# A two-block feed-forward kernel: the second block's first product as seven block products, its weights and their sums prepared in DRAM, its slopes on GpSimd

## The chip, the cores and the metric

One core of one Trainium2 chip. The metric is the device time of one execution in microseconds (us). The engines are called PE (TensorE), DVE (VectorE), ACT (ScalarE), POOL (GpSimd) and SP (SyncE, which only issues transfers here).

## The reference

```python
X = np.fft.fft(np.fft.fft(x, axis=1), axis=2).real        # x: 2 x 3008 x 256
x = X.reshape(6016, 256)
h = x @ w_in                                               # 256 -> 2048
g = np.where(h > 0, h, np.exp(np.minimum(h, 0)) - 1)
x = g @ w_out                                              # 2048 -> 256
h = x @ w_in2                                              # second block, 256 -> 2048
g = np.maximum(h, 0) + alpha * np.minimum(h, 0)            # alpha: one slope per feature
return g @ w_out2                                          # 2048 -> 256
```

## The kernel before

Every product of the two blocks is made of three matmuls in fp32r: each operand is split into a high part and a low rest, and high x high, high x low and low x high are added up in PSUM.

Tokens run in NT = 6 tiles of up to 1024 columns, a plus half of TW = 512 and a minus half of 512 (384 in the last tile). The 2048 hidden features run in NF = 16 slices of 128. A step is one slice of one tile; there are S1 = 96 steps in each block, and PE interleaves two jobs in each: the up product of step s and the down product of step s - 3.

- First block: `up1` is 7 matmuls (the Fourier transform is folded into the weights W1). ACT copies one half (`copy_q`), DVE combines the halves into H (`combine`, two instructions), ACT and DVE form the activation (`neg`, `exp_neg`, `elu`), ACT rounds it to Gh (`g_hi`, L481), DVE takes the rest Gl (`g_lo`, L625). `down1` is 12 matmuls into ACC, which holds the four output blocks in four PSUM banks. In the middle of tiles 0 to 4, `flip2` makes the inputs of the next tile.
- Between the blocks the result of each tile goes to DRAM (`y_scratch`) and comes back as `y_in`, which is split into `y_hl`, for tile 0 by ACT and DVE in four pieces at slices 9 to 12 of the first block's last tile.
- Second block: `up2` (L380 to L382) is 12 matmuls: 2 input blocks of 128, times the plus and the minus half, times three. ACT takes the positive part and the negated negative part from PSUM (`second`, L542 and L544), DVE adds the slope times the negative part (`prelu`, L617), then `g_hi` (L483), `g_lo` (L627) and the 12 matmuls of `down`. At slice 2 of each tile ACT and DVE copy the last tile's ACC out.

Everything is written out by hand: each engine's list is in program order and waits on semaphores. PE's up product of step s waits until the PSUM half of step s - 2 has been read, and its down product for `lo_ready`, which DVE's `g_lo` gives.

POOL splits the weights. Each piece of 512 columns is loaded to `raw`, its high part is one `tensor_scalar` (L265), its rest one `tensor_tensor` (L266). W2's 8 pieces run at the start; the 8 pieces of W3 and 8 of W4 (the second block's weights) wait for the last `flip2` (their place is T1's) and then for one `down_done` each, so they run beside the last tiles of the first block:

```python
if k > after_w2:
    gp.wait_ge(down_done, NF * (LAST - 1) + FLIP_AT - 2 + W34_PACE * (k - after_w2))
```

Of the kernel before, what the change touches and what calls it, by code (L numbers as in the profile page):

```python
# [8 lines left out]
PT = 128  # L9
# [28 lines left out]
def program(nc, x, wa, wb, w2, w3, w4, alpha, c47, cw, cf, out):  # L38
# [4 lines left out]
    y_dram = nc.dram_tensor("y_scratch", [NT, PT, YW], fp32).ap()  # L43

# [13 lines left out]
    y_hl = at("y_hl", o1, [PT, 2 * 2 * YW], f32r)  # L58
    W1_HALF = 2 * YW // (4 * PT)
# [4 lines left out]
    W4 = at("W4", o2, [PT, 2, NF * D], f32r)  # L64
    W3h = at("W3h", o2 + 32 * KB, [PT, ND * F], f32r)
# [19 lines left out]
    W3l = at("W3l", o5, [PT, ND * F], f32r)  # L85
# [9 lines left out]
    with ExitStack() as ctx:  # L95
# [14 lines left out]
        w34_ready = sem("w34_ready")  # L110
# [10 lines left out]
        half_done = sem("half_done")  # L121
        y0h_ready, yh_ready, yl_ready = sem("y0h_ready"), sem("yh_ready"), sem("yl_ready")
# [19 lines left out]
        def _(sp):  # L142
# [68 lines left out]
        def _(gp):  # L211
            n = [0]

            def chain(ins):
                n[0] += 1
                ins.then_inc(pool_step, 1)
                gp.wait_ge(pool_step, n[0])
# [12 lines left out]
            gp.wait_ge(alpha_in, 16)  # L230
            chain(gp.tensor_scalar(nalpha[:, :], alpha_sb[:, :], -1.0, 0.0, ALU.mult, ALU.add))

            pieces = []

            def add(src, hi, lo):
                for c in range(src.shape[1] // 512):
                    sl = slice(c * 512, (c + 1) * 512)
                    pieces.append((src[:, sl], hi[:, sl], lo[:, sl]))

            add(w2, W2[:, 0, :], W2[:, 1, :])  # L240
            after_w2 = len(pieces)
            add(w3, W3h, W3l)
            add(w4, W4[:, 0, :], W4[:, 1, :])

            def load(k):
                gp.dma_start(raw[:, k % 2, :], pieces[k][0]).then_inc(raw_in[k % 2], 16)

            gp.wait_ge(f1_done, 2 * 6)
            load(0)
            load(1)  # L250
# [8 lines left out]
            for k, (_, hi, lo) in enumerate(pieces):  # L259
                if k == after_w2:  # L260
                    gp.wait_ge(f2_done, NT)
                if k > after_w2:
                    gp.wait_ge(down_done, NF * (LAST - 1) + FLIP_AT - 2 + W34_PACE * (k - after_w2))
                gp.wait_ge(raw_in[k % 2], 16 * (k // 2 + 1))
                chain(gp.tensor_scalar(hi, raw[:, k % 2, :], 1.0, 0.0, ALU.mult, ALU.add))  # L265
                ins = gp.tensor_tensor(lo, raw[:, k % 2, :], f32(hi), ALU.subtract)  # L266
                ready = w2_ready if k < after_w2 else w34_ready
                ins.then_inc(ready, 1)
                gp.wait_ge(ready, k + 1 if k < after_w2 else k + 1 - after_w2)
                if k + 2 < len(pieces):  # L270
                    load(k + 2)

        @block.tensor
        def _(pe):
# [87 lines left out]
            def up2(t, f, m):  # L362
                s = NF * t + f
                j = f % 2
                if f == 0:
                    pe.wait_ge(yl_ready, 2 * t + 2)
                if s < 2:
                    pe.wait_ge(comb_ready, S1 + s - 1)
                else:
                    pe.wait_ge(act_ready, S1 + s - 1)  # L370

                def mov(hl, k, w):
                    o = t % 2 * 2 * YW + hl * YW + k * TW
                    return y_hl[:, o:o + w]

                for sign, w in ((0, TW), (1, m)):
                    o = PQ[:, j, sign * TW:sign * TW + w]
                    for c in range(ND):
                        sl = slice(c * F + f * PT, c * F + (f + 1) * PT)
                        mm(o, W3h[:, sl], mov(0, sign * ND + c, w), start=c == 0, stop=False)  # L380
                        mm(o, W3h[:, sl], mov(1, sign * ND + c, w), start=False, stop=False)  # L381
                        ins = mm(o, W3l[:, sl], mov(0, sign * ND + c, w), start=False, stop=c == ND - 1)  # L382
                ins.then_inc(up_done, 1)

            def down(s, W):
# [6 lines left out]
                for d in range(ND):  # L392
                    sl = slice(f * D + d * PT, f * D + (d + 1) * PT)
                    for sign, w in ((0, TW), (1, m)):
                        o = ACC[:, sign * ND + d, 0:w]
                        c = sign * TW
                        mm(o, W[:, 0, sl], Gh[:, j, c:c + w], start=f == 0, stop=False)  # L397
                        mm(o, W[:, 0, sl], Gl[:, j, c:c + w], start=False, stop=False)  # L398
                    for sign, w in ((0, TW), (1, m)):
                        o = ACC[:, sign * ND + d, 0:w]  # L400
                        c = sign * TW
                        ins = mm(o, W[:, 1, sl], Gh[:, j, c:c + w], start=False, stop=f == NF - 1)  # L402
                    if s == 2 * S1 - 1 and d < ND - 1:
                        ins.then_inc(half_done, 1)
                ins.then_inc(down_done, 1)

            def down1(s):
                if s < NF and s % 2 == 0:
                    pe.wait_ge(w2_ready, s // 2 + 1)
                down(s, W2)  # L410

            def down2(s):
                down(s, W4)

# [12 lines left out]
            pe.wait_ge(w34_ready, 16)  # L427
            for f in range(3):
                up2(0, f, TW)
                down1(S1 - 3 + f)  # L430
            for s in range(3, S1):
                up2(s // NF, s % NF, width(s) - TW)
                down2(S1 + s - 3)
            for s in range(S1 - 3, S1):
                down2(S1 + s)

        @block.scalar
        def _(act):
# [36 lines left out]
            def g_hi(s, bias):  # L475
                j, n = s % 2, width(s)
# [27 lines left out]
            def y0_split_hi(k):  # L504
                act.wait_ge(y_loaded, 16)
                act.wait_ge(up_done, S1 - NF + W1_HALF)
                fn(y_hl[:, k * TW:(k + 1) * TW], y_in[:, k * TW:(k + 1) * TW], ACT.Copy).then_inc(y0h_ready, 1)

            eo_hi(0)
            copy_q(0)  # L510
            for s in range(S1):
# [13 lines left out]
                if t == LAST and f in SPLIT_AT:  # L525
                    y0_split_hi(SPLIT_AT.index(f))

            def y_split_hi(t, half):
                c = half * ND * TW
                m = TW - SKIP if t == LAST and half else TW  # L530
                if half == 0:
                    act.wait_ge(y_loaded, 16 * t + (32 if t == LAST else 16))
                o = t % 2 * 2 * YW + c
                dst = y_hl[:, o:o + ND * TW].rearrange("p (a b) -> p a b", a=ND)
                src = y_in[:, c:c + ND * TW].rearrange("p (a b) -> p a b", a=ND)
                fn(dst[:, :, 0:m], src[:, :, 0:m], ACT.Copy).then_inc(yh_ready, 1)

            def second(s):
                j, n = s % 2, width(s)
                act.wait_ge(up_done, s + 1)  # L540
                act.wait_ge(g_ready, s - 1)
                fn(H[:, j, 0:n], PQ[:, j, 0:n], ACT.Relu)  # L542
                act.wait_ge(lo_ready, s - 1)
                fn(G[:, j, 0:n], PQ[:, j, 0:n], ACT.Relu, scale=-1.0).then_inc(act_ready, 1)  # L544

            g_hi(S1 - 1, -1.0)
            for s in range(S1, 2 * S1):
                t, f = s // NF - NT, s % NF
                second(s)
                if s > S1:  # L550
                    g_hi(s - 1, None)
                if f in (6, 9) and t < LAST:
                    y_split_hi(t + 1, (f - 6) // 3)
                if f == 2:
                    y_plus(NT + t - 1)
# [7 lines left out]
        def _(dve):  # L563
# [72 lines left out]
            def y0_split_lo(k):  # L636
# [3 lines left out]
                if k % 2:  # L640
                    ins.then_inc(yl_ready, 1)
# [119 lines left out]
```

## Time and profile before

| | us |
|---|---|
| median of 3 runs | 1018.0 (1017.17 to 1018.95) |
| the profiled execution | 1018.47 |
| its span | 1016.7 |
| PE busy | 999.1 (98%) |
| ACT busy | 655.6 (64%) |
| DVE busy | 632.0 (62%) |
| POOL busy | 89.2 (9%) |

Matmul rows are pipelined: a row of 0.39 us starts while the one before it still runs, so PE's rate is read from the distance of the starts. The first block's steps run from about 58 us to 489 us of the span, the second's from there to the end.

### The profile page before, as it was taken

How to read it: one execution, taken by the hardware profiler on the slowest of the kernel's cores; microseconds unless marked ns; L12 is line 12 of the kernel's file. 1: busy time of each engine (PE TensorE's matmuls, PEld its weight loads, DVE VectorE, ACT ScalarE, POOL GpSimd, SP SyncE). 2: the span in 40 equal slices, each digit the busy share in tenths (PEclk: the TensorE clock that was granted, in tenths of full speed). 3: DMA queues.
4: the chain of work that ended last, by engine and by line, in shares of the span. 5: the costliest groups of instructions: out<-in, count | busy, mean ns of one | idle time of the engine just before them, and what ended most of it. 6: DMA issues, size and time to landing. Idle time of an engine off the chain costs nothing.

```text
span 1016.7 us, 11653 instructions
## 1 busy us (share of the span) xinstructions
PE 999.1 (98%) x4610; PEld 832.2 (82%) x4610; DVE 632.0 (62%) x640; ACT 655.6 (64%) x733; POOL 89.2 (9%) x95
## 2 busy tenths in 40 slices
PE   7979999999999999999999999999999999999997
PEld 6868888888888888878888888888888888888886
DVE  3357887887887887899645445445545545544443
ACT  2247887887787787778766566565555655565554
POOL 3370000000000005860000000000000000000000
PEclk9979999999999999999999999999999999999999
DMA  9420010010010010230020020010002002000101
GB/s 241 132 83 1 1 42 1 1 41 1 1 42 1 1 42 32 63 135 0 1 78 1 1 83 1 1 51 33 0 1 83 1 1 78 1 1 0 42 1 42
DMA packets 8482, 34.59 MB, mean 34 GB/s; under 512 B 1338, under 2 KB 2042, under 8 KB 6508
## 3 DMA queue, kind: packets, MB, share of 16 engines
q1 hardware_dynamic: 5612, 25.03, 7.4%
q0 software_dynamic: 2816, 8.82, 2.9%
q8 instruction: 36, 0.59, 0.2%
q14 instruction: 18, 0.15, 0.1%
HBM read 21.34 MB, written 12.48 MB: 33 GB/s over the span
## 4 chain that ended last, share of the span: by engine, by line
PE 59%; DVE 1%; ACT 0%; issue 0%; DVEq 0%; ACTq 0%
PE ACC L397 11%; PE ACC L402 10%; PE ACC L398 10%; PE PQ L382 8%; PE PQ L381 8%; PE PQ L380 8%; DVE Gl L625 1%; PE PQ L353 0%; PE PQ L354 0%; PE PQ L359 0%; PE PQ L355 0%; PE PQ L358 0%; PE PQ L360 0%; PE PQ L357 0%; DVE H L607 0%; DVE Gl L627 0%
## 5 line engine op out<-in xcount | busy, mean ns | idle before, releaser
L397 PE MATMUL ACC<-Gh,W 128*128 128x512 f32 (+1 forms) x768 | 298.7, 389 | 3.8 <-DVE Gl L625 2.8
L398 PE MATMUL ACC<-Gl,W 128*128 128x512 f32 (+1 forms) x768 | 297.0, 387 | 0.0
L627 DVE TENSOR_TENSOR Gl<-G,Gh 128x1024 fp32r<-128x1024 f32 (+1 forms) x96 | 115.5, 1203 | 214.6 <-ACT Gh L483 214.6
L402 PE MATMUL ACC<-Gh,W 128*128 128x512 f32 (+1 forms) x768 | 234.7, 387 | 0.0
L542 ACT ACTIVATE H<-PQ 128x1024 f32<-128x1024 f32 (+1 forms) x96 | 97.1, 1011 | 131.0 <-PE PQ L382 131.0
L397 PEld LDWEIGHTS ACC<-Gh,W 128*128 128x128 f32 x768 | 144.7, 188 | 38.1 <-issue 4.4
L398 PEld LDWEIGHTS ACC<-Gl,W 128*128 128x128 f32 x768 | 144.8, 188 | 28.0
L402 PEld LDWEIGHTS ACC<-Gh,W 128*128 128x128 f32 x768 | 144.0, 188 | 25.4
L483 ACT ACTIVATE Gh<-G 128x1024 fp32r<-128x1024 f32 (+1 forms) x96 | 100.1, 1042 | 75.2 <-PE ACC L402 71.5
L382 PE MATMUL PQ<-y_hl,W3l 128*128 128x512 f32 (+1 forms) x384 | 147.9, 385 | 0.0
L381 PE MATMUL PQ<-y_hl,W3h 128*128 128x512 f32 (+1 forms) x384 | 147.9, 385 | 0.0
L380 PE MATMUL PQ<-y_hl,W3h 128*128 128x512 f32 (+1 forms) x384 | 147.8, 385 | 0.0
L625 DVE SCALAR_TENSOR_TENSOR Gl<-G,Gh 128x1024 fp32r<-128x1024 f32 (+1 forms) x96 | 116.4, 1213 | 32.8 <-ACT Gh L481 32.4
L612 DVE SCALAR_TENSOR_TENSOR G<-H,G 128x1024 f32<-128x1024 f32 (+1 forms) x96 | 122.4, 1275 | 0.5 <-ACT G L502 0.5
L617 DVE SCALAR_TENSOR_TENSOR G<-G,nalpha,H 128x1024 f32<-128x1024 f32 (+1 forms) x96 | 120.7, 1257 | 0.7 <-ACT G L544 0.7
L473 ACT ACTIVATE Qs<-PQ 128x512 f32<-128x512 f32 x96 | 57.3, 597 | 83.2 <-PE PQ L355 83.2
L481 ACT ACTIVATE Gh<-G 128x1024 fp32r<-128x1024 f32 (+1 forms) x96 | 99.2, 1033 | 9.1 <-DVE G L612 6.6
L497 ACT ACTIVATE G<-H 128x1024 f32<-128x1024 f32 (+1 forms) x96 | 99.5, 1037 | 4.1 <-DVE Gl L625 3.4
L544 ACT ACTIVATE G<-PQ 128x1024 f32<-128x1024 f32 (+1 forms) x96 | 96.3, 1003 | 7.0 <-DVE Gl L627 7.0
L502 ACT ACTIVATE G<-G 128x1024 f32<-128x1024 f32 (+1 forms) x96 | 99.1, 1032 | 0.0
L606 DVE TENSOR_TENSOR H<-PQ,Qs 128x512 f32<-128x512 f32 x96 | 66.4, 692 | 40.2 <-PE PQ L360 37.3
L380 PEld LDWEIGHTS PQ<-y_hl,W3h 128*128 128x128 f32 x384 | 72.1, 188 | 14.6
(70 smaller groups left out, 922.5 us busy)
## 6 DMA issues: line engine op xcount, KB each, us to landing
xr<-in_x SPq DMA_DIRECT2D x16, 384.0 KB, 4.2
raw<-in_w POOLq DMA_DIRECT2D x24, 256.0 KB, 3.1
y_scratch<-y_st SPq DMA_DIRECT2D x5, 1024.0 KB, 3.9
y_in<-y_scratch SPq DMA_DIRECT2D x5, 1024.0 KB, 8.2
out_y<-y_st SPq DMA_DIRECT2D x5, 1024.0 KB, 5.8
wn<-in_wa POOLq DMA_DIRECT2D x4, 256.0 KB, 11.0
wn<-in_wb POOLq DMA_DIRECT2D x4, 256.0 KB, 11.7
out_y<-y_st SPq DMA_DIRECT2D x2, 512.0 KB, 3.3
```

Source lines behind the costliest of these rows:

```text
L380: mm(o, W3h[:, sl], mov(0, sign * ND + c, w), start=c == 0, stop=False)
L381: mm(o, W3h[:, sl], mov(1, sign * ND + c, w), start=False, stop=False)
L382: ins = mm(o, W3l[:, sl], mov(0, sign * ND + c, w), start=False, stop=c == ND - 1)
L397: mm(o, W[:, 0, sl], Gh[:, j, c:c + w], start=f == 0, stop=False)
L398: mm(o, W[:, 0, sl], Gl[:, j, c:c + w], start=False, stop=False)
L402: ins = mm(o, W[:, 1, sl], Gh[:, j, c:c + w], start=False, stop=f == NF - 1)
L483: fn(Gh[:, j, 0:n], G[:, j, 0:n], ACT.Copy).then_inc(hi_ready, 1)
L497: fn(G[:, j, 0:n], H[:, j, 0:n], ACT.Relu, scale=-1.0).then_inc(neg_ready, 1)
L612: stt(G[:, j, 0:n], H[:, j, 0:n], 0.0, G[:, j, 0:n], ALU.max, ALU.add).then_inc(g_ready, 1)
L617: stt(G[:, j, 0:n], G[:, j, 0:n], nalpha[:, f:f + 1], H[:, j, 0:n], ALU.mult, ALU.add).then_inc(g_ready, 1)
L625: stt(Gl[:, j, 0:n], G[:, j, 0:n], bias, f32(Gh[:, j, 0:n]), ALU.add, ALU.subtract).then_inc(lo_ready, 1)
L627: tt(Gl[:, j, 0:n], G[:, j, 0:n], f32(Gh[:, j, 0:n]), ALU.subtract).then_inc(lo_ready, 1)
```

## The change

The tile's input is seen as 2 x 2 blocks (two input blocks, plus and minus half) and the weights of two slices as a 2 x 2 block matrix, so the second block's up products of two slices are one 2 x 2 by 2 x 2 block product. Before, this was 8 block products of 3 matmuls; now it is 7 (Winograd's form), on sums and differences of blocks. A loop pass (`pair`) now handles two slices; there are 48 pairs.

- PE. `pair(n)` issues 7 `product`s (3 matmuls each) and 8 quarters of `down` (3 matmuls each) in a written order. The products are accumulated in three banks, and two partial sums travel: ACT copies bank_a into bank_b in PSUM (the seed), and bank_b twice into SBUF (`u2`, `u3`).
- ACT, per pair: the seed, `u2`, `u3` and two copies of results into H (c11, c21), 512 wide each, and two `g_hi`. Before: four 1024-wide activations and two `g_hi`.
- DVE, per pair: two 512-wide adds from PSUM and u2 or u3 into H (c22, c12), two `join`s (max(H,0) + G, 1024 wide) in place of two `prelu`s, two `g_lo`.
- POOL, per pair: two `slope`s, G = min(H, 0) * alpha, 1024 wide, which the joins wait for.
- The operands of later tiles (`YS`, seven of them, each in two parts): four differences and seven rests on DVE, seven high parts on ACT, spread over pairs 1 to 7 of the tile before; the whole `y_hl` split is gone. Tile 0's operands are made by POOL alone beside the last tile of the first block. ACC is copied out in four 512-wide pieces.
- The weights. POOL forms W3's four sums and seven splits for two pairs at a time (18 instructions of 512 columns, four times) and W4's splits (16), paced by `up_done` from step 4 of the first block on, 4 instructions to 3 steps, staged in SBUF and stored in DRAM (7 MB and 4 MB). After the last `flip2` they are loaded from DRAM, W3 and three slices of W4 by POOL's queue, the rest of W4 over W2 by SP's queue as W2's slices are done with.

```diff
+W3_FROM = 4
+W4_A = 3
+W4_CUTS = (3, 6, 10, 13, 16)
...
+            def pace():
+                gp.wait_ge(up_done, W3_FROM + steps[0] * 3 // 4)
+                steps[0] += 1
...
+                if u:
+                    gp.wait_ge(w3_stored, 16 * u)
+                pace()
+                chain(gp.tensor_tensor(f32(lo[4]), a21, a22, ALU.add))
...
+                for q, src in ((0, a11), (1, a12), (3, a22), (2, f32(lo[2])), (4, f32(lo[4])), (5, f32(lo[5])), (6, f32(lo[6]))):
+                    pace()
+                    chain(hi_of(hi[q], src))
+                    pace()
+                    chain(gp.tensor_tensor(lo[q], src, f32(hi[q]), ALU.subtract))
+                gp.dma_start(w3_dram[:, 2 * u:2 * u + 2, :, :, :], f32(stage[:, :, :, :, :])).then_inc(w3_stored, 16)
...
+            def parts0(q, src):
+                gp.wait_ge(up_done, NF * LAST + 2 * Y0_ORDER.index(q) + 2)
+                chain(hi_of(ys0(q, 0), src))
+                gp.tensor_tensor(ys0(q, 1), src, f32(ys0(q, 0)), ALU.subtract).then_inc(y0_ready, 1)
...
+            def slope(s):
...
+                if k == 0:
+                    gp.wait_ge(c21_ready, n + 1)
+                    gp.wait_ge(c22_ready, n + 1)
+                else:
+                    gp.wait_ge(c11_ready, n + 1)
+                    gp.wait_ge(c12_ready, n + 1)
+                gp.wait_ge(lo_ready, s - 1)
+                gp.tensor_scalar(G[:, k, 0:w], H[:, k, 0:w], 0.0, alpha_sb[:, f:f + 1], ALU.min, ALU.mult).then_inc(slope_ready, 1)
...
-            def up2(t, f, m):
...
+            def product(n, q, bank, w, start):
...
+                mm(o, w3(p, q, 0), hi, start=start, stop=False, skip_group_check=True)
+                mm(o, w3(p, q, 0), lo, start=False, stop=False, skip_group_check=True)
+                mm(o, w3(p, q, 1), hi, start=False, stop=True, skip_group_check=True).then_inc(p_done[q], 1)
...
+            def pair(n):
+                a, b = S1 + 2 * n - 3, S1 + 2 * n - 2
...
+                product(n, 0, bank_a, TW, True)
...
+                product(n, 4, bank_e(n), m, True)
+                down(a, 0)
+                down(a, 1)
+                pe.wait_ge(seed_ready, n + 1)
+                product(n, 5, bank_b, TW, False)
+                product(n, 1, bank_a, TW, False)
+                down(a, 2)
+                pe.wait_ge(u2_ready, n + 1)
+                product(n, 6, bank_b, TW, False)
+                down(a, 3)
+                down(b, 0)
+                pe.wait_ge(u3_ready, n + 1)
+                product(n, 3, bank_b, TW, False)
+                down(b, 1)
+                down(b, 2)
+                pe.wait_ge(c22_ready, n + 1)
+                product(n, 2, bank_e(n), m, False)
+                down(b, 3)
...
+            for n in range(NT * NP):                       # ACT
...
+                fn(bank_b, bank_a, ACT.Copy).then_inc(seed_ready, 1)
+                if n:
+                    g_hi(S1 + 2 * n - 2, None)
...
+                fn(u2[:, :], bank_b, ACT.Copy).then_inc(u2_ready, 1)
...
+                fn(H[:, 1, 0:TW], bank_a, ACT.Copy).then_inc(c11_ready, 1)
...
+                fn(u3[:, :], bank_b, ACT.Copy).then_inc(u3_ready, 1)
...
+                g_hi(S1 + 2 * n - 1, None if n else -1.0)
...
+                fn(H[:, 0, 0:TW], bank_b, ACT.Copy).then_inc(c21_ready, 1)
...
+                if n:                                      # DVE
+                    join(S1 + 2 * n - 1)
+                    g_lo(S1 + 2 * n - 2, None)
...
+                tt(H[:, 0, TW:TW + m], bank_e(n)[:, 0:m], u3[:, 0:m], ALU.add).then_inc(c22_ready, 1)
+                g_lo(S1 + 2 * n - 1, None if n else -1.0)
...
+                tt(H[:, 1, TW:TW + m], bank_e(n)[:, 0:m], u2[:, 0:m], ALU.add).then_inc(c12_ready, 1)
+                join(S1 + 2 * n)
```

(The comments ACT and DVE in the diff are added here to tell the two lists apart.)

## Rows read from the trace of the kernel before

**Rows 1.** The page's first part: busy time, share of the span, instructions of an engine.
```profile
PE 999.1 (98%) x4610; PEld 832.2 (82%) x4610; DVE 632.0 (62%) x640; ACT 655.6 (64%) x733; POOL 89.2 (9%) x95
```

**Rows 2.** The head of the chain that ended last: shares of the span.
```profile
PE 59%; DVE 1%; ACT 0%; issue 0%; DVEq 0%; ACTq 0%
```

**Rows 3.** Timeline of a first-block step: start us, duration us, engine, line, operation.
```profile
331.20 0.39 PE L353 MATMUL PQ<-EO,W 128*128 128x512 f32 x1
...
332.56 0.39 PE L360 MATMUL PQ<-EO,W1e 128*128 128x512 f32 x1
...
332.99 0.69 DVE L606 TENSOR_TENSOR H<-PQ,Qs 128x512 f32<-128x512 f32 x1 [0.33 <-PE PQ L360]
...
334.61 1.23 DVE L625 SCALAR_TENSOR_TENSOR Gl<-G,Gh 128x1024 fp32r<-128x1024 f32 x1 [0.33 <-ACT Gh L481]
...
335.51 0.39 PE L353 MATMUL PQ<-EO,W 128*128 128x512 f32 x1
```

**Rows 4.** Timeline of PE, second block, a full step's first matmul and the next step's.
```profile
614.10 0.39 PE L380 MATMUL PQ<-y_hl,W3h 128*128 128x512 f32 x1
...
619.54 0.39 PE L380 MATMUL PQ<-y_hl,W3h 128*128 128x512 f32 x1
```

**Rows 5.** Timeline of PE, last tile: first wide, first narrow, end of an up product.
```profile
998.68 0.40 PE L380 MATMUL PQ<-y_hl,W3h 128*128 128x512 f32 x1
...
1000.08 0.33 PE L380 MATMUL PQ<-y_hl,W3h 128*128 128x384 f32 x1
...
1001.13 0.39 PE L397 MATMUL ACC<-Gh,W 128*128 128x512 f32 x1
```

**Rows 6.** Groups by line: shapes and count, busy us, mean ns, idle before, releasers.
```profile
L627 DVE TENSOR_TENSOR Gl<-G,Gh 128x1024 fp32r<-128x1024 f32 (+1 forms) x96 | 115.5, 1203 | 214.6 <-ACT Gh L483 214.6
...
L483 ACT ACTIVATE Gh<-G 128x1024 fp32r<-128x1024 f32 (+1 forms) x96 | 100.1, 1042 | 75.2 <-PE ACC L402 71.5 <-DVE G L617 3.7
...
L612 DVE SCALAR_TENSOR_TENSOR G<-H,G 128x1024 f32<-128x1024 f32 (+1 forms) x96 | 122.4, 1275 | 0.5 <-ACT G L502 0.5
...
L473 ACT ACTIVATE Qs<-PQ 128x512 f32<-128x512 f32 x96 | 57.3, 597 | 83.2 <-PE PQ L355 83.2
```

**Rows 7.** Timeline of POOL at the start: a small, a one-input, a two-input instruction.
```profile
21.92 0.20 POOL L231 TENSOR_SCALAR nalpha<-alpha_sb 128x16 f32<-128x16 f32 x1 [11.91 <-DMA alpha_sb<-in_alpha]
...
48.62 0.61 POOL L265 TENSOR_SCALAR W<-raw 128x512 fp32r<-128x512 f32 x1
49.32 1.27 POOL L266 TENSOR_TENSOR W<-raw,W 128x512 fp32r<-128x512 f32 x1
```

**Rows 8.** Timeline in the first block's last tile: POOL, then DVE.
```profile
457.27 2.01 POOL L266 TENSOR_TENSOR W<-raw,W 128x512 fp32r<-128x512 f32 x1
...
458.04 2.18 DVE L612 SCALAR_TENSOR_TENSOR G<-H,G 128x896 f32<-128x896 f32 x1
...
462.43 1.08 DVE L612 SCALAR_TENSOR_TENSOR G<-H,G 128x896 f32<-128x896 f32 x1
```

**Rows 9.** Timeline of ACT there: `copy_q` once a step, the last without POOL.
```profile
457.47 0.57 ACT L473 ACTIVATE Qs<-PQ 128x512 f32<-128x512 f32 x1
461.96 0.58 ACT L473 ACTIVATE Qs<-PQ 128x512 f32<-128x512 f32 x1
466.04 0.60 ACT L473 ACTIVATE Qs<-PQ 128x512 f32<-128x512 f32 x1 [0.69 <-PE PQ L355]
```

**Rows 10.** Timeline where the blocks meet: first second-block matmul, last `exp_neg`.
```profile
489.61 0.40 PE L380 MATMUL PQ<-y_hl,W3h 128*128 128x512 f32 x1
...
491.73 0.94 ACT L502 ACTIVATE G<-G 128x896 f32<-128x896 f32 x1
```

**Rows 11.** Timeline of the end: last `g_lo` and the down product behind it.
```profile
1008.02 1.09 DVE L627 TENSOR_TENSOR Gl<-G,Gh 128x896 fp32r<-128x896 f32 x1 [1.02 <-ACT Gh L483]
...
1009.17 0.50 PE L397 MATMUL ACC<-Gh,W 128*128 128x512 f32 x1 [0.43 <-DVE Gl L627]
```

**Rows 12.** Transfers: issues, KB each, median us from issue to landing.
```profile
y_in<-y_scratch SPq DMA_DIRECT2D x5, 1024.0 KB, 8.2
```

More of the change, by code:

```diff
@@ L229, in _, with load_w2 @@
             chain(gp.memset(f32(W1e[:, :]), 0.0))
[L230 to L246, printed above, removed]
+            W2_LOADS = NF * D // 512
+            def load_w2(k):
+                gp.dma_start(raw[:, k % 2, :], w2[:, k * 512:(k + 1) * 512]).then_inc(raw_in[k % 2], 16)
             gp.wait_ge(f1_done, 2 * 6)
-            load(0)
-            load(1)
+            load_w2(0)
+            load_w2(1)
             gp.wait_ge(w1l_ready, 8)
@@ L257, in _, with hi_of @@
             gp.memset(f32(W1[0:1, :, 2:4, :]), 0.0).then_inc(w1_ready, 1)
[L259 to L263, printed above, removed]
-                gp.wait_ge(raw_in[k % 2], 16 * (k // 2 + 1))
[L265 to L271, printed above, removed]
+            def hi_of(dst, src):
+                return gp.tensor_scalar(dst, src, 1.0, 0.0, ALU.mult, ALU.add)
@@ new lines, in _ @@
+            for k in range(W2_LOADS):
+                gp.wait_ge(raw_in[k % 2], 16 * (k // 2 + 1))
+                src = raw[:, k % 2, :].rearrange("p (f d) -> p f d", d=D)
+                fs = slice(2 * k, 2 * k + 2)
+                chain(hi_of(W2[:, fs, 0, :], src))
+                gp.tensor_tensor(W2[:, fs, 1, :], src, f32(W2[:, fs, 0, :]), ALU.subtract).then_inc(w2_ready, 1)
+                gp.wait_ge(w2_ready, k + 1)
+                if k + 2 < W2_LOADS:
+                    load_w2(k + 2)
@@ new lines, in _ @@
+            gp.wait_ge(w3_stored, 16 * NP // 2)
+            for v in range(4):
+                for j in range(2):
+                    o = (2 * v + j) * 512
+                    gp.dma_start(raw[:, j, :], w4_in[:, o:o + 512]).then_inc(raw_in[j], 16)
+                loads += 1
+                if v:
+                    gp.wait_ge(w4_stored, 16 * v)
+                for j in range(2):
+                    gp.wait_ge(raw_in[j], 16 * loads)
+                    src = raw[:, j, :].rearrange("p (f d) -> p f d", d=D)
+                    pace()
+                    chain(hi_of(stage4[:, 2 * j:2 * j + 2, 0, :], src))
+                    pace()
+                    chain(gp.tensor_tensor(stage4[:, 2 * j:2 * j + 2, 1, :], src, f32(stage4[:, 2 * j:2 * j + 2, 0, :]), ALU.subtract))
+                gp.dma_start(w4_dram[:, 4 * v:4 * v + 4, :, :], f32(stage4[:, :, :, :])).then_inc(w4_stored, 16)
@@ new lines, in _, with ys0 @@
+            gp.wait_ge(f2_done, NT)
+            for n in range(3):
+                gp.dma_start(f32(W3a[:, 2 * n:2 * n + 2, :, :, :]), w3_dram[:, 2 * n:2 * n + 2, :, :, :]).then_inc(w3_loaded[n], 16)
+            gp.wait_ge(w4_stored, 64)
+            gp.dma_start(f32(W4a[:, :, :, :]), w4_dram[:, 0:W4_A, :, :]).then_inc(w4a_loaded, 16)
+            gp.dma_start(f32(W3b[:, :, :, :, :]), w3_dram[:, NP - 2:NP, :, :, :]).then_inc(w3_loaded[3], 16)
+            def ys0(q, part):
+                return YS[0][q][:, part, :]
@@ new lines, in sum0 @@
+            def sum0(q, a, b):
+                gp.wait_ge(up_done, NF * LAST + 2 * Y0_ORDER.index(q) + 2)
+                chain(gp.tensor_tensor(YT[0][q][:, :], a, b, ALU.subtract))
+            def parts0(q, src):
+                gp.wait_ge(up_done, NF * LAST + 2 * Y0_ORDER.index(q) + 2)
+                chain(hi_of(ys0(q, 0), src))
+                gp.tensor_tensor(ys0(q, 1), src, f32(ys0(q, 0)), ALU.subtract).then_inc(y0_ready, 1)
+            gp.wait_ge(y_loaded, 16)
+            parts0(0, y_block(1, 1))
@@ L360, in up1, with down1 @@
                 mm(o, W1e[:, f * PT:(f + 1) * PT], eo(t, 4), start=False, stop=True).then_inc(up_done, 1)
-            def up2(t, f, m):
[L363 to L385, printed above, removed]
+            def product(n, q, bank, w, start):
+                t, p = n // NP, n % NP
+                if p == 0:
+                    if t:
+                        pe.wait_ge(ysl_ready, NQ7 * (t - 1) + YS_ORDER.index(q) + 1)
+                    else:
+                        pe.wait_ge(y0_ready, Y0_ORDER.index(q) + 1)
+                hi, lo = YS[t % 2][q][:, 0, 0:w], YS[t % 2][q][:, 1, 0:w]
+                o = bank[:, 0:w]
+                mm(o, w3(p, q, 0), hi, start=start, stop=False, skip_group_check=True)
+                mm(o, w3(p, q, 0), lo, start=False, stop=False, skip_group_check=True)
+                mm(o, w3(p, q, 1), hi, start=False, stop=True, skip_group_check=True).then_inc(p_done[q], 1)
+            def down1(s):
+                if s < NF and s % 2 == 0:
+                    pe.wait_ge(w2_ready, s // 2 + 1)
                 f, j = s % NF, s % 2
@@ L401, in down @@
                         c = sign * TW
-                        ins = mm(o, W[:, 1, sl], Gh[:, j, c:c + w], start=False, stop=f == NF - 1)
-                    if s == 2 * S1 - 1 and d < ND - 1:
-                        ins.then_inc(half_done, 1)
+                        ins = mm(o, W2[:, f, 1, sl], Gh[:, j, c:c + w], start=False, stop=f == NF - 1)
                 ins.then_inc(down_done, 1)
[L407 to L410, printed above, removed]
@@ L412, in down2, with down @@
-            def down2(s):
-                down(s, W4)
+            def down(s, g):
+                j, d, sign = s % 2, g // 2, g % 2
+                if g == 0:
+                    pe.wait_ge(lo_ready, s + 1)
+                if s < S1:
+                    W, first, last, w = W2[:, s % NF, :, :], False, s == S1 - 1, (TW, WL - TW)[sign]
+                else:
+                    n, i = (s - S1) // 2, (s - S1) % NF
+                    f = 2 * (n % NP) + 1 - i % 2
+                    W, first, last, w = w4_slice(f), i == 0, i == NF - 1, (TW, minus(n))[sign]
+                    if n < NP and g == 0 and f < W4_A:
+                        pe.wait_ge(w4a_loaded, 16)
+                    if n < NP and g == 0 and f >= W4_A:
+                        pe.wait_ge(w4_loaded[[f < c for c in W4_CUTS[1:]].index(True)], 16)
+                    if first and sign == 0:
+                        pe.wait_ge(accp_ready, 2 * (n // NP) + d + 1)
+                    if first and sign == 1:
+                        pe.wait_ge(accm_ready, 2 * (n // NP) + d + 1)
+                c = sign * TW
+                o = ACC[:, sign * ND + d, 0:w]
+                sl = slice(d * PT, (d + 1) * PT)
+                mm(o, W[:, 0, sl], Gh[:, j, c:c + w], start=first, stop=False)
+                mm(o, W[:, 0, sl], Gl[:, j, c:c + w], start=False, stop=False)
+                ins = mm(o, W[:, 1, sl], Gh[:, j, c:c + w], start=False, stop=last)
+                if g == 3:
+                    ins.then_inc(down_done, 1)
+                elif last:
+                    ins.then_inc(acc_done, 1)
@@ L426, in _ @@
                     down1(s - 3)
[L427 to L435, printed above, removed]
+            for n in range(NT * NP):
+                pair(n)
+            for s in range(2 * S1 - 3, 2 * S1):
+                for g in range(4):
+                    down(s, g)
         @block.scalar
@@ L538, in second, with acc_plus @@
[L538 to L555, printed above, removed]
+            def acc_plus(n, d):
+                act.wait_ge(acc_done, 3 * (n - NT + 1) + 2 * d + 1)
+                act.wait_ge(y_stored, y_free(n))
+                fn(y_st[:, 0, d, :], ACC[:, d, :], ACT.Copy).then_inc(accp_ready, 1)
@@ L556, in _ @@
+            g_hi(2 * S1 - 2, None)
             g_hi(2 * S1 - 1, None)
-            act.wait_ge(y_stored, y_free(2 * NT - 1))
             for d in range(ND):
-                act.wait_ge(half_done, 1) if d < ND - 1 else act.wait_ge(down_done, 2 * S1)
-                fn(y_st[:, 0, d, :], ACC[:, d, :], ACT.Copy).then_inc(yp_ready, 1)
+                acc_plus(2 * NT - 1, d)
         @block.vector
```

294 lines of the change are left out of this document (216 added, 78 removed).

## The prediction

> **What bounds the kernel now.** I read the page's busy shares first: PE is busy for 98% of the span, ACT and DVE for under two thirds [rows 1]. A pipelined matmul counts as busy, so this alone could hide a slow rhythm. The chain that ended last says the same from the other side: its named work is PE's, 59% (the pieces of the pipelined matmuls), against 1% of DVE [rows 2]. Third, the timeline: a second-block step starts 5.44 us after the one before, for 24 matmuls of 512 columns, 0.2267 us each [rows 4]; in the last tile an up product's 6 wide matmuls take 1.40 us and its 6 narrow ones 1.05, so 0.233 and 0.175 each [rows 5]. A first-block step takes 4.31 us for 19 matmuls, again 0.2267 [rows 3]. PE's matmul count is the bound in both blocks, so each matmul that goes is worth its 0.2267 us, as long as the other engines keep up.
>
> **What goes.** A pair of slices took 48 matmuls and takes 45. In five tiles that is 40 pairs x 3 x 0.2267 = 27.2 us. In the last tile a pair had 24 wide and 24 narrow matmuls, 9.79 us; five of the seven products are now wide, so it has 27 and 18, 9.44 us: 0.35 x 8 = 2.8 us. Together 30.0 us.
> POOL's old W3 and W4 splits go from the first block's last tile. There a step took 4.49 us beside them and 4.08 once they had ended [rows 9]: DVE's `elu` needed 2.18 us in place of 1.08, and POOL's rest 2.01 in place of 1.27 [rows 7, 8]. Five such steps: 2.0 us back. The ACT and DVE split of tile 0 also goes; those steps ran at 4.08, so nothing.
>
> **Does a pair run at PE's rate?** This is the choice that decides. I lay a full pair out by durations of rows. PE has 15 groups of 0.68 us, 10.2 us in all. A group's last result is seen by another engine 0.88 us after the group's start: 2 x 0.2267, then 0.39, then 0.04 [rows 3]. A 512-wide ACT copy takes 0.60, `g_hi` 1.04, `g_lo` 1.20 [rows 6]; an add from PSUM 0.69 [rows 3]; a join is `elu`'s form, 1.22 without POOL (1.275 on average, rows 6). `slope` is in no row. A one-input POOL instruction takes 0.61 for 512 columns and 0.20 for 16 [rows 7], so 1.04 for 1024; with two inputs 1.27, so (1.27 - 0.20) x 2 + 0.20 = 2.34. These are its ends; it has one tensor input, so I take 1.04.
> - P0 is done at 0.9, the seed at 1.5; P5 needs it at 2.72. P5 is done at 3.6, u2 at 4.2; P6 needs it at 4.76. P1 is done at 4.3, c11 at 4.9. P6 at 5.6, u3 at 6.25; P3 needs it at 6.8. c22 at 7.0; P2 needs its bank at 8.84. P3 at 7.7, c21 at 8.3. The least margin is 0.5 us.
> - The long way round: P2 is done at 9.72. c12 ends at 10.4; the join of k = 0 runs to 11.5, since its slope ended near 9.6 (it waits for c21 and for `g_lo` to leave); the slope of k = 1 can read only behind that join, to 12.6; the join of k = 1 to 13.8; `g_lo` of k = 0 to 15.0. PE wants it at group 9 of the next pair, 10.2 + 6.1 = 16.3. Margin 1.2 us.
> ACT has 3.0 + 2.1 = 5.1 us of work and DVE 2.4 + 2.4 + 1.4 = 6.2, of 10.2. The seven operands of the next tile add at most three 0.69 us instructions to one pair; DVE then reaches c22 near 7.5, done by 8.2, before 8.84. So nothing here costs, and 30 us stand.
> What I took from rows here is that DVE and POOL exclude each other: the row at 458.04 has `elu` waiting for the whole of POOL's `tensor_tensor` [rows 8]. The Trainium skill (SBUF — State Buffer, section "Who interferes with whom") calls this an exclusive lock between a DVE instruction with two SBUF inputs and a GpSimd one that reads SBUF; the trace agrees (2.18 us against 1.08). By a reading without it the slope would run beside the join and the margin would be 2.2 us, with the same sum.
>
> **What the new form adds.**
> - POOL's 88 instructions in the first block (44 in the sums and rests of W3 with two inputs, 28 with one, 16 for W4), 4 to 3 steps, mean 1.0 us. They wait for `up_done`, which also starts `combine`, an instruction pair with one SBUF input, 1.3 us, with 0.33 us idle behind it [rows 3]. A single one of 1.27 fits into 1.6 us. Two in a row (every third step) overrun by 0.4 us, two with two inputs by 1.0; DVE idles 0.66 us per step, and `g_lo` ends 1.2 us before PE's next down product (334.61 + 1.23 against 335.51 + 1.6), so PE does not see it. After the eight stores POOL is behind and runs without its pacing; a few steps may cost 0.4 each, as in rows 9. I take 1 us, between -1 (nothing was lost before either) and 18 (the second rival).
> - Tile 0's operands on POOL: 18 instructions, 11 x 1.27 + 7 x 0.61 = 18 us over 14 steps, in four bursts of over 3 us. By 0.41 us for each burst: 1.5 us, between 0 and 5.
> - The seam. P5 of pair 0 needs the seed, which stands behind the last `exp_neg` on ACT: that ended at 492.67, the seed at 493.3, and P5 would be due at 489.61 + 2.6 = 492.2 [rows 10]. 1.1 us.
> - Tile ends. In a tile's second pair ACT has two more copies of 0.6 and DVE two of 0.69 and a difference; `g_lo` of k = 1 ends near 9.2, the last piece of ACC at 9.9, and PE wants that bank at group 14, 9.52. 0.4 us x 6 = 2.4, between 0 and 6.
> - The end. Behind the last pair the long way round has 2.45 us of down product (two wide quarters of 0.70, two narrow of 0.52) to hide it. In narrow durations (1.09 for `g_lo`, rows 11) it ends at 13.9 after a pair start, and PE is there at 9.44 + 2.45 = 11.9: 2.0 us idle, where 0.43 was idle before [rows 11]. 1.5 us.
> - Transfers: W3 and W4 come back as 11 MB after the last `flip2`. At 8.2 us for 1 MB [rows 12], which holds the latency too, that is 90 us for all of it, and the 8 MB on POOL's queue 66 us, from 387 to 453; the first pair starts at 489. Hidden behind tiles 4 and 5; if that cover failed, it would be a plain wait at 489.
> - `load_y` of tile 1 is queued on SP behind the last piece of W4, issued near 490. Both are 1.8 MB, 15 us, landed by 505; DVE asks for it in pair 1, near 507. Nothing, but 5 us if tile 0's operands come late: what is queued behind that DVE instruction is c22, for which PE waits.
>
> **Sum.** -30.0 - 2.0 + 1.0 + 1.5 + 1.1 + 2.4 + 1.5 = -24.5 us. The profiled execution of 1018.47 us (span 1016.7 and 1.8 around it) becomes 994.0; the median of the runs lies 0.5 lower: 993.5. I say 994.
>
> **The rivals.**
> - GpSimd becomes the bound, slower than before. If `slope` costs x, DVE's first join starts at 10.3 or at 8.6 + x, whichever is later, and the long way round ends x + 3.6 us after that. It is free up to x = 2.0. With the two-input price, x = 2.34, it ends at 16.9, 0.6 us late in each of 48 pairs: 29 us, 1023. From x = 2.3 on the change loses. For it: no row has a per-feature factor and a minimum on POOL. Against it: one tensor input, and the copy form had two operations as well. The Trainium skill speaks for it: GPSIMD Engine Reference, "Performance versus the Vector engine", gives 2.6 cycles at 1.2 GHz for each element of a two-input instruction, an estimate of 2.2 us for 1024, and advises against elementwise work there; its 1.8 cycles for a tight loop would be 1.5 us, which fits the margin. The row of 0.61 us for 512 is faster than either.
> - The first block falls out of step. In rows 9 a late POOL made DVE late, and DVE made the next POOL instruction late, for five steps. If that held over the 66 steps of the weight work, with 4/3 instead of 2 instructions a step, it costs 66 x 0.41 x 2/3 = 18 us: 1011. For it: DVE has 0.66 us a step to spare. Against it: beside the full tile 4 the old splits ran without loss, and `up_done` is a better moment than `down_done`.
> - The seams cost more: tile 0's operands and the load of tile 1 late, ACC's pieces late by 1 us. 5 + 1 + 4 us more: about 1003.
> - All additions are hidden: -30.0 - 2.0, 986.
>
> **How the numbers follow.** Forecast (989 to 999) 0.62; seams 0.12; first block out of step, wholly or in part (1000 to 1013), 0.12; everything hidden 0.06; GpSimd's slope between free and decisive (1000 to 1016) 0.02, deciding 0.06. A measurement of this kernel tells from no change only what is over 0.2%, 2 us. Faster is all but the last and some of the worst mixes: 0.90; within 0.2% 0.03; slower 0.07. The range reaches from 988, near the hidden case, to 1009, into the second rival, and leaves out about 2 in 10.
>
> **What will show it.** PE: 4466 matmuls; second-block pairs 10.2 us apart, 9.44 in the last tile; a wider distance names the rival, and the idle time before PE's products and downs says which way round was late. POOL: `slope` near 1.04 us. First block: step distances of 4.31 us between 75 and 430 us of the span, and the first product at 489.6 give or take 2 us. Seams: PE idle once near 492, six times about 0.4, and 2 us before the last but one down product. The prediction is wrong if pairs are over 10.4 us apart or if the second block starts after 500.

## The result and the profile after

The change made the kernel slower: 1161.5 us (median of 4 runs, 1158.8 to 1166.0) against 1017.6 (the kernel before, now with a fourth run), a ratio of 1.142 (95% interval 1.1385 to 1.1456). I had said 994.

The page's first part and its slices of POOL's busy tenths and of PE's granted clock, after the change; the span is 1160.2 us:

```profile
PE 1023.8 (88%) x4466; PEld 826.0 (71%) x4466; DVE 712.6 (61%) x783; ACT 606.9 (52%) x808; POOL 563.7 (49%) x278
...
POOL 3461313123155006256666666665566666565563
PEclk9999999999999999989999998989999989899898
```

The head of the chain that ended last:

```profile
POOL 24%; PE 24%; DVE 9%; issue 8%; ACT 1%; POOLq 0%; DVEq 0%; ACTq 0%
```

PE issues the 4466 matmuls that were forecast, 144 fewer than in [rows 1], yet its busy share fell from 98% to 88%, and POOL now has as large a part (24%) as PE of a chain that was PE's [rows 2]. The groups by line name the instruction (columns as in rows 6):

```profile
L424 POOL TENSOR_SCALAR G<-H,alpha_sb 128x1024 f32<-128x1024 f32 (+1 forms) x96 | 407.1, 4249 | 262.5 <-ACT H L767 222.8 <-DVE H L931 34.7 <-DVE Gl L852 4.8
...
L842 DVE SCALAR_TENSOR_TENSOR G<-H,G 128x1024 f32<-128x1024 f32 (+1 forms) x96 | 115.5, 1203 | 239.5 <-POOL G L424 239.2
L582 PE MATMUL ACC<-Gh,W 128*128 128x512 f32 x324 | 139.9, 432 | 101.2 <-DVE Gl L852 101.2
```

Read upward: PE's down product waits 101 us for `g_lo`, the joins wait 239 us for `slope`, and one `slope` takes 4.25 us on average. One loop in the timeline, ACT, POOL, DVE and PE merged from it by me in order of start (a POOL row that merges the two slopes stands first, the second slope alone behind it):

```profile
716.38 0.60 ACT L767 ACTIVATE H<-PQ 128x512 f32<-128x512 f32 x1 [2.03 <-PE PQ L536]
...
717.07 8.53 POOL L424 TENSOR_SCALAR G<-H,alpha_sb 128x1024 f32<-128x1024 f32 x2 [6.11 <-ACT H L767]
...
720.81 1.23 DVE L842 SCALAR_TENSOR_TENSOR G<-H,G 128x1024 f32<-128x1024 f32 x1
720.86 4.75 POOL L424 TENSOR_SCALAR G<-H,alpha_sb 128x1024 f32<-128x1024 f32 x1
...
725.64 1.23 DVE L842 SCALAR_TENSOR_TENSOR G<-H,G 128x1024 f32<-128x1024 f32 x1 [3.60 <-POOL G L424]
726.78 1.22 DVE L852 TENSOR_TENSOR Gl<-G,Gh 128x1024 fp32r<-128x1024 f32 x1
...
728.05 0.50 PE L582 MATMUL ACC<-Gh,W4a 128*128 128x512 f32 x1 [1.26 <-DVE Gl L852]
```

The second slope starts 3.79 us behind the first; a slope that waits for nothing reads 3.71 us. The second one reads 4.75: it waits about 1.05 us for the first join, which starts beside it. The same holds in all 48 pairs (4.75 to 4.77 us in the full tiles). This is the long way round of the prediction, with another price for one of its steps. The seeds' starts (one seed in each pair) lie 13.62 us apart on average over the second block (640.4 us for 47 distances), where 10.2 was forecast, and 9.44 in the last tile.

The first block went as forecast in its steps, not in its end. Steps stayed at 4.31 us; its last tile ran at 4.08 with three steps of 4.60, 4.43 and 4.60 beside tile 0's operands (1.4 us; I had 1.5), and the five slow steps of [rows 9] are gone. The second block began at 485.0 us, which lies outside the 489.6 give or take 2 that I had named; in the later runs of the same first block it began between 484.5 and 489.5. Most of the difference arises at the very start: the first four steps took 13.7 us here and 16.1 in e1 below, whose first block is the same code.

### The profile page after: what moved, and what is told of

Its sections match the earlier page's. It is cut to its first block, busy times and chain, and to the rows that moved or that the text cites. A ratio compares the mean times of both kernels' runs of the same rounds, so it can differ in the third digit from the quotient of the medians.

```text
span 1160.2 us, 12203 instructions
## 1 busy us (share of the span) xinstructions
PE 1023.8 (88%) x4466; PEld 826.0 (71%) x4466; DVE 712.6 (61%) x783; ACT 606.9 (52%) x808; POOL 563.7 (49%) x278
## 4 chain that ended last, share of the span: by engine, by line
POOL 24%; PE 24%; DVE 9%; issue 8%; ACT 1%; POOLq 0%; DVEq 0%; ACTq 0%
POOL G L424 24%; DVE Gl L852 5%; PE ACC L582 4%; PE ACC L583 3%; PE ACC L584 3%; PE PQ L536 2%; PE PQ L534 2%; PE PQ L535 2%; DVE H L936 2%; PE ACC L552 1%; PE ACC L557 1%; PE ACC L553 1%; DVE Gl L850 1%; DVE YS L892 0%; ACT H L767 0%
## 5 line engine op out<-in xcount | busy, mean ns | idle before, releaser
L424 POOL TENSOR_SCALAR G<-H,alpha_sb 128x1024 f32<-128x1024 f32 (+1 forms) x96 | 407.1, 4249 | 262.5 <-ACT H L767 222.8
L842 DVE SCALAR_TENSOR_TENSOR G<-H,G 128x1024 f32<-128x1024 f32 (+1 forms) x96 | 115.5, 1203 | 239.5 <-POOL G L424 239.2
L582 PE MATMUL ACC<-Gh,W 128*128 128x512 f32 x324 | 139.9, 432 | 101.2 <-DVE Gl L852 101.2
L582 PEld LDWEIGHTS ACC<-Gh,W 128*128 128x128 f32 x324 | 66.6, 206 | 130.7 <-DVE Gl L852 118.5
L552 PE MATMUL ACC<-Gh,W 128*128 128x512 f32 x372 | 145.5, 391 | 3.5 <-DVE Gl L850 3.5
L553 PE MATMUL ACC<-Gl,W 128*128 128x512 f32 x372 | 144.4, 388 | 0.0
L850 DVE SCALAR_TENSOR_TENSOR Gl<-G,Gh 128x1024 fp32r<-128x1024 f32 (+1 forms) x96 | 120.0, 1250 | 28.5 <-ACT Gh L688 27.9
L583 PE MATMUL ACC<-Gl,W 128*128 128x512 f32 x324 | 134.0, 414 | 0.0
L584 PE MATMUL ACC<-Gh,W 128*128 128x512 f32 x324 | 133.7, 413 | 0.0
L837 DVE SCALAR_TENSOR_TENSOR G<-H,G 128x1024 f32<-128x1024 f32 (+1 forms) x96 | 123.7, 1288 | 0.6 <-ACT G L709 0.6
L557 PE MATMUL ACC<-Gh,W 128*128 128x512 f32 x372 | 113.9, 387 | 0.0
L534 PE MATMUL PQ<-YS,W3a 128*128 128x512 f32 (+1 forms) x252 | 104.3, 414 | 8.1 <-ACT u L754 7.0
L757 ACT ACTIVATE H<-PQ 128x512 f32<-128x512 f32 x48 | 28.7, 597 | 141.6 <-DVE G L842 141.5
L535 PE MATMUL PQ<-YS,W3a 128*128 128x512 f32 (+1 forms) x252 | 101.9, 404 | 0.0
L536 PE MATMUL PQ<-YS,W3a 128*128 128x512 f32 (+1 forms) x252 | 101.7, 404 | 0.0
L746 ACT ACTIVATE PQ<-PQ 128x512 f32<-128x512 f32 x48 | 27.9, 582 | 128.9 <-PE PQ L536 128.9
```

The lines of the kernel that those rows point to most:

```text
L424: gp.tensor_scalar(G[:, k, 0:w], H[:, k, 0:w], 0.0, alpha_sb[:, f:f + 1], ALU.min, ALU.mult).then_inc(slope_ready, 1)
L534: mm(o, w3(p, q, 0), hi, start=start, stop=False, skip_group_check=True)
L535: mm(o, w3(p, q, 0), lo, start=False, stop=False, skip_group_check=True)
L536: mm(o, w3(p, q, 1), hi, start=False, stop=True, skip_group_check=True).then_inc(p_done[q], 1)
L552: mm(o, W2[:, f, 0, sl], Gh[:, j, c:c + w], start=f == 0, stop=False)
L553: mm(o, W2[:, f, 0, sl], Gl[:, j, c:c + w], start=False, stop=False)
```

## The experiments

The first four ask what makes the slope slow, and what the kernel is without it. e1 to e3 edit one line of the changed kernel; e4 takes `slope` off POOL and changes `join`. In the cuts below G and H stand for G[:, k, 0:w] and H[:, k, 0:w], and the semaphore at the end of a line is left out; where only a + line is shown, its - line is that of e1. A time without a ratio is that of a single run; the changed kernel's four runs spread over 7 us.

**e1_const**, a constant for the factor:
```diff
-gp.tensor_scalar(G, H, 0.0, alpha_sb[:, f:f + 1], ALU.min, ALU.mult)
+gp.tensor_scalar(G, H, 0.0, 0.15, ALU.min, ALU.mult)
```


> The changed kernel with the slope's per-feature factor replaced by one constant, 0.15 (the slopes are then not the reference's); minimum and multiplication stay. Theory A, the minimum is what makes the slope 4.25 us: it stays near 4.25 us, pairs near 13.8 us apart, time near 1160. Theory B, the factor read from SBUF makes it: the slope falls to 1.0 to 1.5 us, pairs to 10.2 us, time near 989 (second block from 485.0, 40 x 10.2 + 8 x 9.44, 1.1 + 2.4 + 1.5 of seams, 13.3 of end, 1.8 outside the span). Theory C, the slope waits for DVE's lock or is slow wherever it stands: near 4.25 us here and in the two kernels beside it.

1088.9 us, pairs 12.07 apart. The slope still takes 3.6 us, so B falls as the main cause. The time fell by 73 us all the same; e12 and what follows it take that up.

**e2_ptr**, the factor without the minimum:
```diff
+gp.tensor_scalar(G, H, alpha_sb[:, f:f + 1], 0.0, ALU.mult, ALU.add)
```


> The changed kernel with the slope as H times the per-feature factor plus 0, no minimum (so positive values are counted with their slope too; not the reference's activation). Theory A: the slope falls to 1.0 to 1.5 us, pairs 10.2 us apart, time near 989. Theory B: it stays near 4.25 us, time near 1160. Theory C: 4.25 us.

989.7 us, pairs 10.20. A holds: it is the minimum. (Mean 1.61 us per slope, waits for DVE in it.)

**e3_muladd**, neither:
```diff
+gp.tensor_scalar(G, H, 0.15, 0.0, ALU.mult, ALU.add)
```


> The changed kernel with the slope as H times 0.15 plus 0: no minimum, no factor from SBUF, the form of POOL's copies (not the reference's activation). Theories A and B: 1.0 to 1.1 us (0.61 for 512 columns), pairs 10.2 us apart, time near 989. Theory C: 4.25 us. If A and B both hold a part, this one alone is fast and the other two lie between.

988.5 us. C falls: the place in the program and the waits for DVE cost nothing in PE's time. The seeds' 47 distances add up to 474.3 us against 640.4: 166.1 of the 173.5 us between the two spans (1160.2 and 986.7); the rest is the end, 9.6 longer, and a start 2.2 earlier.

**e4_dve**, the slope on DVE, inside the join:
```diff
-stt(G[:, k, 0:w], H[:, k, 0:w], 0.0, G[:, k, 0:w], ALU.max, ALU.add)
+stt(G[:, k, 0:w], H[:, k, 0:w], alpha_sb[:, f:f + 1], H[:, k, 0:w], ALU.mult, ALU.max)
```


> The changed kernel with no slope on POOL: DVE's join is one instruction, max(alpha x H, H), the same as the reference's for every slope up to 1. If POOL's slope alone cost the time (A, B or C), each pair keeps PE busy: 10.2 us apart, 9.44 in the last tile, time 986 to 990, ratio to before near 0.97. The rival, that the seven-product form has a second bound of its own (ACT's five copies, the seed, the pieces of ACC), says pairs of 10.6 us or more and 1005 or more.

987.7 us, ratio to before 0.9705 (0.9683 to 0.9727); pairs 10.20 and 9.41. No second bound shows: the pairs run at PE's rate. Its chain is PE's again:

```profile
PE 58%; DVE 2%; ACT 1%; issue 0%; DVEq 0%; ACTq 0%
```

The next four ask which minimum is slow: any, or one order of operations.

**e5_swap**, factor first:
```diff
+gp.tensor_scalar(G, H, alpha_sb[:, f:f + 1], 0.0, ALU.mult, ALU.min)
```


> The changed kernel with the slope's two operations in the other order: H times the per-feature factor first, then the minimum with 0. The same function. Theory A1, any minimum is slow on POOL: slope near 3.7 us and time near 1160. Theory A2, only a pair of operations whose first is not the multiplication is slow (the one fast form seen so far multiplies first): 1.1 us without waits, time near 989.

**e6_max**, a maximum:
```diff
+gp.tensor_scalar(G, H, 0.0, 0.15, ALU.max, ALU.mult)
```


> The changed kernel with a maximum with 0 in place of the minimum, and the constant 0.15 as factor (not the reference's slopes). A1, widened to comparisons: 3.6 us, time near 1089 as with the minimum and a constant. If only the minimum itself is slow: 1.1 us and 989.

**e7_addmul**, another order of two plain operations:
```diff
+gp.tensor_scalar(G, H, 0.0, 0.15, ALU.add, ALU.mult)
```


> The changed kernel with the slope as (H + 0) times 0.15: no comparison, the multiplication second (the minimum is left out). A1: 1.1 us without waits, time near 988. A2: 3.6 us, time near 1089.

**e8_minonly**, one operation:
```diff
+gp.tensor_scalar(G, H, 0.0, None, ALU.min)
```


> The changed kernel with only the minimum with 0 in the slope, one operation, no factor (so negative values count fully). A1: still about 3.6 us if the price is of the minimum, time near 1089; if the price is of a pair of unlike operations, 1.1 us and 988.

1143.1, 1086.4, 989.7 and 1014.4 us. A2 falls (e7 is fast, e5 slow), A1 holds, for the maximum too. A lone minimum lies between, which neither theory had: 2.77 us. e5 came out 17 us under the 1160 expected, with the same price for a slope; why is taken up behind e12. What in POOL makes a minimum dear, no run shows. Lines and instructions of 128 columns in the order after, e1, e3, e6, e8 (ns: least, median, largest; the least are the 896-wide ones, without waits):

```profile
L424 POOL TENSOR_SCALAR G<-H,alpha_sb x96: 3274/4376/4774, 494.3 to 1142.3; 128x1024 f32<-128x1024 f32 x80, 128x896 f32<-128x896 f32 x16
```
```profile
L424 POOL TENSOR_SCALAR G<-H x96: 3193/3628/4478, 498.0 to 1070.8; 128x1024 f32<-128x1024 f32 x80, 128x896 f32<-128x896 f32 x16
```
```profile
L424 POOL TENSOR_SCALAR G<-H x96: 952/1603/1909, 496.4 to 973.3; 128x1024 f32<-128x1024 f32 x80, 128x896 f32<-128x896 f32 x16
```
```profile
L424 POOL TENSOR_SCALAR G<-H x96: 3196/3626/4477, 495.4 to 1068.1; 128x1024 f32<-128x1024 f32 x80, 128x896 f32<-128x896 f32 x16
```
```profile
L424 POOL TENSOR_SCALAR G<-H x96: 2445/2772/3619, 498.7 to 997.1; 128x1024 f32<-128x1024 f32 x80, 128x896 f32<-128x896 f32 x16
```

So 896 columns take 0.95 us with multiply and add, 2.45 with a minimum alone, 3.19 with a minimum or maximum and a multiplication; the factor from SBUF adds 0.06 to 0.08 (e2 and the changed kernel).

**e9_twice** tests the schedule's margin, a plain slope done twice:
```diff
+chain(gp.tensor_scalar(G, H, 0.15, 0.0, ALU.mult, ALU.add))
+gp.tensor_scalar(G, H, 0.15, 0.0, ALU.mult, ALU.add)
```


> The kernel with H times 0.15 plus 0 as slope (no minimum, constant factor), each slope computed twice, the second after the first: one slope then takes about 2 x 1.07 + 0.1 = 2.24 us where it took 1.07. It tests the schedule of the prediction, by which a slope is free up to 2.0 us: the long way round ends at 10.84 + 2.24 + 3.6 = 16.7 against 16.3, 0.35 us late in each of 48 pairs, 17 us more than the single one's 988.5: about 1005, pairs 10.55 us apart. If the margin were wider than the schedule has it, 990 or less; if the lock made POOL lose more, above 1015.

999.4 us, 11 more than the single one, where about 17 more was expected. Most pairs stay at 10.2; two of each tile, those with three more DVE instructions for the next operands, take 11.0. The margin of plain pairs was wider than 16.7 against 16.3 said; that of the loaded ones was too small.

**e10_tail** swaps two calls at the end of e4:
```diff
-            join(2 * S1 - 1)
             g_lo(2 * S1 - 2, None)
+            join(2 * S1 - 1)
```


> The version with the slope in DVE's join, and behind the last pair the rest of k = 0 computed before the join of k = 1. PE's idle time before the last but one down product (0.85 us) should fall to nothing and that before the last one come in its place, at most 0.4: about 0.5 us less than the 987.7 of the version without, which a comparison of times can hardly tell. Ratio to before 0.970.

986.6 us, ratio 0.9709 (0.9684 to 0.9734). Not told apart from e4, and the idle time it was meant to take away stayed at 0.85 us, with 0.47 more before the last product: ACT's `g_hi` sets it, not DVE's order. My reason for it was wrong.

**e11_before_dve** is the control, the kernel before with e4's slope (ACT's two activations become one copy):
```diff
-fn(G[:, j, 0:n], PQ[:, j, 0:n], ACT.Relu, scale=-1.0)
...
+stt(G[:, j, 0:n], H[:, j, 0:n], alpha_sb[:, f:f + 1], H[:, j, 0:n], ALU.mult, ALU.max)
```


> The kernel before, eight block products, with only its slopes changed: ACT copies the up product to H in one instruction, DVE forms max(alpha x H, H). PE bound it already, so the same time as before within 0.2% (1015 to 1019); then the 29 us of the version with seven products and the slope on DVE are the products' and not the slope form's. If the slope form itself helped, under 1013.

1017.0 us, ratio 0.9999 (0.9985 to 1.0013). So the 29 us of e4 are not the slope form's; they belong to the seven products and what was moved with them.

**e12_warm** takes up what the slope's price leaves open. In full tiles, the first distance left out, pairs of the changed kernel came 11.8 to 16.4 us apart, e1's 12.0 to 13.0, for slopes whose prices differ by 0.08 us. Two stretches of the changed kernel, behind an idle time of 2.65 us and after (us; busy and count of PE, PEld, DVE, ACT, POOL; granted clock; DMA):

```profile
713.40:719.50 6.10, 6.08 (x14) 4.84 (x15) 1.92 (x2) 1.54 (x3) 2.43 (x1) 0.50 0.00 0
719.50:726.40 6.90, 6.90 (x31) 5.65 (x30) 2.68 (x3) 2.72 (x4) 6.02 (x2) 0.99 0.00 0
```

Granted clock 0.50 is TensorE's lower level, 1.2 GHz: 14 matmuls in 6.1 us, then 31 in 6.9. PE stood idle once in each pair, mostly for 1.3 to 2.65 us; the clock fell in 20 of the 47 distances between seeds, 78 us in all. In full tiles 17 such distances were 15.1 us on average and the other 22 were 13.0. e12 puts discarded matmuls into that idle time:

```diff
                 down(a, 3)
+                if n:
+                    pe.wait_ge(c12_ready, n)
+                    for _ in range(9):
+                        mm(bank_e(n + 1), w3(p, 0, 0), YS[t % 2][0][:, 0, 0:TW], start=True, stop=True, skip_group_check=True)
                 down(b, 0)
```


> The changed kernel with nine more matmuls in each pair, 2.04 us, into the bank that is free then, just ahead of the down product that waits for the slopes; their results are thrown away. In the changed kernel PE stood idle 2.65 us there and then ran its next 14 matmuls 0.43 us apart at a lower granted clock, and pairs came 13.3 to 15.9 us apart. If those idle times bring the clock down and the clock draws the pairs out, PE now runs at full clock, all pairs take the 13.3 us of the slopes' loop (13.0 to 13.6), and the kernel is faster with more work: about 1140 (40 pairs x 0.5 less), granted clock 0.99. If the spread of the pairs comes from the slopes and DVE's lock alone, the time stays within 1150 to 1165. If the nine matmuls are simply in the way, above 1165.

1144.9 us, 14 us under the least of the four runs of the changed kernel (1158.8), with 423 more matmuls. Its span of 1143.1 has clock 0.995 and, in full tiles, distances of 13.27 to 14.30, 13.29 in most pairs. All 48 second slopes wait for the join here too, so the clock is what differs. From 500 to 900 us, the changed kernel first:

```profile
500.00:900.00 400.00, 326.55 (x1289) 253.28 (x1289) 203.49 (x223) 155.44 (x237) 248.95 (x58) 0.94 0.05 19
```
```profile
500.00:900.00 400.00, 375.15 (x1587) 292.46 (x1585) 207.11 (x227) 158.23 (x243) 256.26 (x59) 1.00 0.05 19
```

What it leaves is 13.29 against e1's 12.04. With the constant, the join is the one that waits, and reads 2.05 us:

```profile
650.57 3.63 POOL L424 TENSOR_SCALAR G<-H 128x1024 f32<-128x1024 f32 x1
650.64 2.05 DVE L842 SCALAR_TENSOR_TENSOR G<-H,G 128x1024 f32<-128x1024 f32 x1 [1.61 <-POOL G L424]
```

The slopes then run back to back and 1.07 us fewer stand in the loop. Who waits can't be read from which row starts first: in e1 and in 45 pairs of the changed kernel alike the slope's row starts ahead, by 0.06 to 0.07 us and by 0.05 to 0.06. e5 has both outcomes in one execution, here a pair of each:

```profile
558.47 3.71 POOL L424 TENSOR_SCALAR G<-H,alpha_sb 128x1024 f32<-128x1024 f32 x1
558.53 2.13 DVE L842 SCALAR_TENSOR_TENSOR G<-H,G 128x1024 f32<-128x1024 f32 x1 [0.30 <-POOL G L424]
...
544.96 4.77 POOL L424 TENSOR_SCALAR G<-H,alpha_sb 128x1024 f32<-128x1024 f32 x1
545.01 1.23 DVE L842 SCALAR_TENSOR_TENSOR G<-H,G 128x1024 f32<-128x1024 f32 x1 [2.67 <-POOL G L424]
```

From one first slope to the next, its eleven full loops of the first kind took 12.20 to 12.35 us, its 28 of the second kind 13.27 or more. In the changed kernel all 48 pairs are of the second kind, in e1 all of the first. That, and the clock at its lower level for 52 us in place of 78, sets e5 apart from the changed kernel and accounts for the 17 us. In the first kind the join waits only 0.9 us and ends while the slope still runs.

So an estimate splits the 166.1 us in four parts, which add up to 167: 93 with e1's price and order (567.3 - 474.3), 7.5 from the factor (0.16 x 47), 50 from the order (1.07 x 47), 16.5 from the clock (640.4 - 623.9, e12's sum).

## Why the prediction was wrong

- *The failed step* is the price of `slope`, "so 1.04 for 1024", with 2.34 as its other end. It measured 3.71 us without waits, 3.79 from its start to the next one's. I took the price from two rows of POOL that multiply and add, and bounded it by the number of inputs; the operation itself, a minimum, was in no row, and my upper end did not cover it. I wrote that no row had "a per-feature factor and a minimum", and gave the case 8%.
- *The mechanism was there*, as the first rival: POOL's slopes, the joins and `g_lo` hold up PE's down product. Its formula is not borne out. It puts a join between the two slopes of every pair, so that the loop is 6.1 + 2x us. With x = 3.79 that is 13.7 a pair, 3.5 us late, 167 us in 48 pairs: 1161, as measured. That this fits is in part luck. It is 13.29 in plain pairs at full clock (e12), and the lower clock, which I had not thought of, gives back about as much. And where the join is the one that waits, the formula is 1.3 us a pair too long: for e1's 3.63 it says 1146 (1088.9 measured), for e8's 2.77 it says 1063 (1014.4). The measured plain loops of e8 and e1, 10.4 and 12.04, are 4.8 + 2x. So "From x = 2.3 on the change loses" is wrong too: at 2.77 the kernel took 1014.4 us against 1017.0 before.
- *PE's rate*: right. Pairs of 10.20 and 9.41 wherever the slope is short (e2, e3, e4). The sum, made for such a slope, was 994.0; e3's profiled execution took 988.5, at the low edge of the range, near the case in which everything is hidden (986). By the sum the second block would begin at 490.1; in e3 it began at 487.2, which is 2.9 of the 5.5 us.
- *The additions*: POOL's weight work cost nothing (1.0 forecast; W3's instructions are 256 columns wide, 0.41 and 0.74 us, and not 512, as the section on the change says and the prediction prices). The seam measured 0.82 us (1.1), tile ends 0.2 each, in e3 and e4 (0.4). At the end PE was idle 1.6 us in e3, with the short slope on POOL (2.0), and 0.85 in e4. "The first block falls out of step" did not occur, nor a late load.
- *DVE and POOL exclude each other*: a wait shows in the short slopes too (e3's second ones read 1.9 us in place of 1.05), and costs nothing there. But a join does not wait for the whole of a long slope, as the row at 458.04 suggested: it waited 0.8 to 0.9 us and ended about 1.5 us before the slope (e1, e5). Which of the two waits decides about 1.1 us per pair.
- The Trainium skill (GPSIMD Engine Reference, section "Engine selection") has one-input elementwise work on GpSimd, maximum among it, as "roughly line-rate". The trace agrees for multiply and add (1.05 us for 1024 columns) and not for maximum, nor for minimum, which the page doesn't name: 3.6 us with a multiplication, where DVE's join of the same width takes 1.23. The measurement decides.

## What to carry to other kernels

Price an instruction by a row with the same operation, not only the same shape and inputs, and where none exists let the upper end be several times the nearest row before moving work into a loop with 1 us of margin. A leaky slope up to 1 is one instruction, max(alpha x H, H); it needs no second engine. And when one engine waits in every loop, count what its clock loses too.

## What was not expected of the hardware

- POOL's minimum (alone, 2.6 times) and its minimum or maximum with a multiplication (3.4 times) cost far more than its multiply and add, at 896 columns.
- With PE idle for 1.3 to 2.65 us once in each pair, its granted clock fell to 0.50 in 20 of 47 pairs; filling 2.04 us of each idle time with discarded matmuls made the kernel about 16 us faster.
- Slope and join start within 0.05 to 0.07 us of each other, and in one kernel (e5) now the one waits and now the other: about 1.1 us of a loop hang on it.
